# Attention copies by whole units, first scores by pairs, and high parts ahead of low parts in a fused attention, expert and mixer kernel

## What is computed

```python
# 1. attention, 8 heads of 64, 768 positions: window of 16, plus one summary key/value per 32 positions
k_sum = k.reshape(B, H, nb, 32, D).max(axis=3); v_sum = v.reshape(B, H, nb, 32, D).mean(axis=3)
scores = concat([where(|i - j| < 16, q @ k.T, -1e9), q @ k_sum.T + log(32)])   # both scaled by 1/8
x = softmax(scores) @ concat([v, v_sum])
# 2. four experts, each a causal attention of width 64 with an output product; the gate keeps two of them
x = sum over the chosen e of w_e * (softmax(causal(x wq_e (x wk_e).T)) @ (x wv_e)) @ wo_e
# 3. mixer: over tokens (768 -> 256 -> 768), then over channels (512 -> 1536 -> 512), each with a residual
u = x + (relu(x.T @ w_tok1) @ w_tok2).T
out = u + relu(u @ w_ch1) @ w_ch2
```

## Time and profile before

| | |
|---|---|
| median of 3 runs | 444.56 us (444.51 to 444.81) |
| profiled execution | 445.28 us |
| span of its trace | 443.4 us |
| TensorE matmuls busy | 429.9 us, 97% |
| TensorE weight loads busy | 365.1 us, 82% |
| VectorE busy | 294.1 us, 66% |
| ScalarE busy | 228.2 us, 51% |
| GpSimd busy | 144.1 us, 33% |

### The profile page before, as it was taken

The page is one execution under the profiler, slowest core; times in us unless marked ns, Lnnn a source line. Parts: engine busy times, 40 slices in busy tenths (PEclk is TensorE's granted clock), DMA queues, the critical chain, the costliest instruction groups (busy, mean ns, idle before and its releaser), DMA issues.

```text
span 443.4 us, 8595 instructions
## 1 busy us (share of the span) xinstructions
PE 429.9 (97%) x3326; PEld 365.1 (82%) x3326; DVE 294.1 (66%) x531; ACT 228.2 (51%) x592; POOL 144.1 (33%) x162
## 2 busy tenths in 40 slices
PE   7889999999999899999999999999999999999996
PEld 3568996887767799978876898998999898889885
DVE  4885469775469725687766985776775775475353
ACT  5885657765249844876865353444442233323120
POOL 5797947000028602000285265433032022200000
PEclk9999999999999999999999999999999999999999
DMA  8954290000671310000034012123113053301103
GB/s 288 343 200 142 78 316 5 1 2 1 237 294 60 112 58 1 0 1 1 2 96 143 0 49 57 46 88 96 47 49 95 37 201 95 94 3 49 47 1 142
DMA packets 14800, 39.67 MB, mean 89 GB/s; under 512 B 1656, under 2 KB 3368, under 8 KB 14760
## 3 DMA queue, kind: packets, MB, share of 16 engines
q1 hardware_dynamic: 14328, 38.60, 26.2%
q10 hardware_dynamic: 432, 0.52, 0.4%
HBM read 33.56 MB, written 4.72 MB: 86 GB/s over the span
## 4 chain that ended last, share of the span: by engine, by line
PE 87%; DVE 7%; ACT 2%; issue 2%; POOL 1%; DVEq 0%; POOLq 0%
PE ps_s L753 34%; PE ps_o L753 20%; PE ps_x L753 15%; PE ps_t L753 11%; PE ps_t L927 4%; PE ps_t L820 2%; ACT PA L1169 1%; DVE X_l L1569 1%; DVE nmaxA L1432 1%; DVE vsum L1599 1%; DVE PTA L1450 1%; PE ps_x L944 1%; ACT KW L1178 1%; DVE denA L1437 0%; POOL PA L595 0%
## 5 line engine op out<-in xcount | busy, mean ns | idle before, releaser
L1411 ACT ACTIVATE HID_h<-HID_raw 128x384 fp32r<-128x384 f32 x48 | 25.2, 526 | 72.3 <-DVE HID_raw L1768 32.2
L698 POOL TENSOR_TENSOR W_raw<-W_raw 128x256 f32<-128x256 f32 x11 | 11.6, 1055 | 99.9 <-DMA W_raw<-in_ch 88.6
L595 POOL TENSOR_TENSOR PA<-PA,denA 128x480 f32<-128x480 f32 x24 | 23.8, 993 | 51.9 <-DVE denA L1443 51.8
L1169 ACT ACTIVATE PA<-ps_s,nmaxA 128x120 f32<-128x120 f32 x96 | 34.1, 391 | 11.5 <-DVE nmaxA L1432 11.4
L753 PE MATMUL ps_s<-C_h,HID_l 128*128 128x512 f32 x96 | 37.7, 393 | 0.0
L753 PE MATMUL ps_s<-C_l,HID_h 128*128 128x512 f32 x96 | 37.7, 393 | 0.0
L753 PE MATMUL ps_s<-C_h,HID_h 128*128 128x512 f32 x96 | 37.6, 392 | 0.0
L1527 DVE TENSOR_REDUCE nmaxM<-ps_s 128x1 f32<-128x640 f32 (+5 forms) x28 | 26.8, 956 | 13.1 <-PE ps_s L753 13.0
L1757 DVE SCALAR_TENSOR_TENSOR HID_l<-HID_raw,HID_h 128x384 fp32r<-128x384 f32 x48 | 28.1, 590 | 10.5 <-ACT HID_h L1411 8.1
L1239 ACT ACTIVATE PM<-ps_s,nmaxM 128x128 f32<-128x128 f32 (+5 forms) x48 | 30.2, 635 | 5.6 <-DVE nmaxM L1527 5.2
L753 PE MATMUL ps_o<-V_h,W_h 128*128 128x384 f32 x96 | 32.8, 342 | 0.1
(11 more groups left out here) (257 smaller groups left out, 1277.6 us busy)
## 6 DMA issues: line engine op xcount, KB each, us to landing
VW<-in_vw SPq DMA_DIRECT2D x12, 512.0 KB, 7.7
W_raw<-in_ch SPq DMA_DIRECT2D x12, 512.0 KB, 3.6
C_raw<-in_ch SPq DMA_DIRECT2D x12, 512.0 KB, 3.9
VT<-in_vT SPq DMA_DIRECT2D x8, 384.0 KB, 7.3
out_x<-US SPq DMA_DIRECT2D x11, 256.0 KB, 2.0
QT<-in_qT SPq DMA_DIRECT2D x7, 384.0 KB, 7.3
KP<-in_kT SPq DMA_DIRECT2D x6, 384.0 KB, 7.1
raw<-in_tok SPq DMA_DIRECT2D x4, 384.0 KB, 3.2
```

The source lines that it names most:

```text
L595: pool.tensor_tensor(PA[:, u % NPA, :, :], PA[:, u % NPA, :, :], denA[:, u % 2, 1, :].unsqueeze(2).broadcast_to([P, 4, KC]), ALU.mult).the ...
L698: pool.tensor_tensor(W[S3], W[A11], W[A21], ALU.subtract).then_inc(w_sum, 1)
L1169: last = act.activation(PA[:, u % NPA, j, :], ps_s[u % 2][:, j % 2, (j // 2) * KC:(j // 2 + 1) * KC], ACT.Exp, bias=nmaxA[:, u % 4, j:j + ...
L1411: act.activation(*own(s, n, half), ACT.Relu).then_inc(g_hi, 1)
```

## The change

1. A unit's four transposes go into one bank of `ps_t` (bank u % 2), 120x512. ScalarE copies even units, VectorE copies odd units, each in one instruction. The transposes of unit u wait for the copy of unit u-2, the values for one engine's copy.
2. The second means get a function of their own in step 8, in bank 0, behind the copy of unit 4; the transposes of unit 6 wait until they are read. The value sums move to steps 5 and 6. ScalarE writes `VS` from PSUM first, and `VW` from `VS` behind a wait on it.
3. First scores: ScalarE fills pair 0's summary behind its first two window copies, VectorE pair 1's only, reducing pair 0's two halves first. The score matmuls wait pair by pair, behind the mask matmuls. There is one more constant matmul before them (12).
4. `m_out_project` and `m_token1` issue all products with the high part of the moving tile first, wait for the low part only then, and issue the products with it last.
5. The values of unit 0 of batch 1 get a wait of their own for the last `add_tokens` (`m_u`).

```diff
-N_WARM = 11
+N_WARM = 12
-SUMS_AT = (6, 7)
-MEANS_AT = 5
+SUMS_AT = (5, 6)
+MEANS_AT = 8
@@ a_scores
-                if t == 0:
-                    pe.wait_ge(*((a_kfill, 2) if b == 1 and q == 0 else (a_kfill0, 2 * (b + q) + 2)))
+                if t == 0 and b + q > 0:
+                    pe.wait_ge(*((a_kfill, 2) if b == 1 and q == 0 else (a_kfill0, 2 * (b + q) + 1)))
...
                     pair = 2 * q + j
+                    if b + u == 0:
+                        pe.wait_ge(*((a_kfirst, 1) if j == 0 else (a_kfill0, 1)))
@@ a_second_means (new), a_transpose, a_values
+            def a_second_means(b):
+                pe.wait_ge(a_pt0, turned(b, MEANS_AT - 4))
+                means(SECOND_MEANS, b, 1).then_inc(a_vm, 1)
...
-                if u >= 1:
-                    pe.wait_ge(a_pt0, b * NU + u)
-                    pe.wait_ge(a_pt1, b * NU + u)
+                if u >= 2:
+                    pe.wait_ge(a_pt1 if u % 2 else a_pt0, turned(b, u - 2))
+                if u == MEANS_AT - 2:
+                    pe.wait_ge(a_vs, 2 * b + 2)
                 for j in range(4):
-                    last = pe.transpose(ps_t[0:KC, j // 2, (j % 2) * P:(j % 2 + 1) * P], PA[:, u % NPA, j, :], ident[:, :])
+                    last = pe.transpose(ps_t[0:KC, u % 2, j * P:(j + 1) * P], PA[:, u % NPA, j, :], ident[:, :])
...
-                pe.wait_ge(a_pt0, b * NU + (u + 1))
-                pe.wait_ge(a_pt1, b * NU + (u + 1))
+                pe.wait_ge(a_pt1 if u % 2 else a_pt0, turned(b, u))
+                if b > 0 and u == 0:
+                    pe.wait_ge(m_u, b * TQ)
@@ m_out_project
-                pe.wait_ge(m_ol, b * TQ + (t + 1))
+                pe.wait_ge(m_oh, b * TQ + (t + 1))
...
+                for k in range(EP):
+                    mm(ps_x[:, :], OT_h[:, k, :], wo_h[:, k, :], k == 0, False)
+                    mm(ps_x[:, :], OT_h[:, k, :], wo_l[:, k, :], False, False)
+                pe.wait_ge(m_ol, b * TQ + (t + 1))
+                for k in range(EP):
+                    last = mm(ps_x[:, :], OT_l[:, k, :], wo_h[:, k, :], False, k == EP - 1)
@@ m_token1
+                pe.wait_ge(m_xh, b * TQ + (t + 1))
+                cols = slice(m * P, (m + 1) * P)
+                mm(bank[2 * m], tok1_h[:, t, cols], X2_h[:, t, :], t == 0, False)
+                mm(bank[2 * m], tok1_l[:, t, cols], X2_h[:, t, :], False, False)
                 pe.wait_ge(m_xl, b * TQ + (t + 1))
+                last = mm(bank[2 * m], tok1_h[:, t, cols], X2_l[:, t, :], False, t == TQ - 1)
@@ scalar: a_means, a_to_sbuf
+                act.activation(VS[WK:KC, q, :], sums, ACT.Copy, scale=1.0 / BLOCK).then_inc(a_vs, 1)
+                act.wait_ge(a_vs, 2 * b + q + 1)
...
-                act.activation(VW[WK:KC, q, 0:n, :], sums.unsqueeze(1).broadcast_to([NB, n, 2 * P]), ACT.Copy,
-                               scale=1.0 / BLOCK).then_inc(a_vd, 1)
-                act.activation(VS[WK:KC, q, :], sums, ACT.Copy, scale=1.0 / BLOCK).then_inc(a_vs, 1)
+                act.activation(VW[WK:KC, q, 0:n, :], VS[WK:KC, q, :].unsqueeze(1).broadcast_to([NB, n, 2 * P]),
+                               ACT.Copy).then_inc(a_vd, 1)
...
-                act.activation(PTA[:, u % 2, 2:4, :].rearrange("p j q -> p (j q)"), ps_t[0:KC, 1, 0:2 * P],
-                               ACT.Copy).then_inc(a_pt1, 1)
+                act.activation(PTA[:, 0, :, :].rearrange("p j q -> p (j q)"), ps_t[0:KC, 0, :], ACT.Copy).then_inc(a_pt0, 1)
@@ vector: a_to_sbuf, start
-                dve.tensor_copy(PTA[:, u % 2, 0:2, :].rearrange("p j q -> p (j q)"),
-                                ps_t[0:KC, 0, 0:2 * P]).then_inc(a_pt0, 1)
+                dve.tensor_copy(PTA[:, 1, :, :].rearrange("p j q -> p (j q)"), ps_t[0:KC, 1, :]).then_inc(a_pt1, 1)
...
             for r in range(2):
-                half_of_key_maxima(r, 0)
-            for r in range(2):
-                half_of_key_maxima(r, 1)
-                fill_maxima(0, r)
+                for half in range(2):
+                    half_of_key_maxima(r, half)
+            fill_maxima(0, 1)
```

More of the change, by code:

```diff
@@ L278, in program @@
         project_bank = [bank[i][:, 0:GS] for i in (3, 0, 1, 2, 4, 5)] + [ps_o[:, 0:GS], ps_x[:, 0:GS]]
-        FIRST_MEANS = [ps_x[:, 0:2 * P]] + [ps_t[:, 1, 2 * P:4 * P]] * (B - 1)
+        FIRST_MEANS = [ps_x[:, 0:2 * P]] + [ps_t[:, 1, 0:2 * P]] * (B - 1)
+        SECOND_MEANS = ps_t[:, 0, 0:2 * P]
         turn_bank = [ps_o[:, :], ps_x[:, :]]
@@ L308, in program @@
         a_zero = sem("a_zero")
-        a_kfill0 = sem("a_kfill0"); a_kfill = sem("a_kfill")
+        a_kfirst = sem("a_kfirst"); a_kfill0 = sem("a_kfill0"); a_kfill = sem("a_kfill")
         a_kwin0 = sem("a_kwin0"); a_kwin = sem("a_kwin")
@@ L396, in load_half_of_keys, with turned @@
                              kT_d[0, :, r * S + cols.start:r * S + cols.stop]).then_inc((ld_kf, ld_k)[half][r], 16)
+        def turned(b, u):
+            return b * NU // 2 + u // 2 + 1
         def u_row(g, j):
@@ L815, in a_transpose @@
                     pe.wait_ge(a_vs, 2 * b + 1)
-                if u >= 1:
-                    pe.wait_ge(a_pt0, b * NU + u)
-                    pe.wait_ge(a_pt1, b * NU + u)
+                if u >= 2:
+                    pe.wait_ge(a_pt1 if u % 2 else a_pt0, turned(b, u - 2))
+                if u == MEANS_AT - 2:
+                    pe.wait_ge(a_vs, 2 * b + 2)
                 for j in range(4):
-                    last = pe.transpose(ps_t[0:KC, j // 2, (j % 2) * P:(j % 2 + 1) * P], PA[:, u % NPA, j, :], ident[:, :])
-                if u == MEANS_AT:
-                    last = means(ps_t[:, 1, 2 * P:4 * P], b, 1)
+                    last = pe.transpose(ps_t[0:KC, u % 2, j * P:(j + 1) * P], PA[:, u % NPA, j, :], ident[:, :])
                 last.then_inc(a_t, 1)
@@ L868, in m_project @@
                 if g == 4:
-                    pe.wait_ge(a_pt0, b * NU + NU)
-                    pe.wait_ge(a_pt1, b * NU + NU)
+                    pe.wait_ge(a_pt0, turned(b, NU - 2))
+                    pe.wait_ge(a_pt1, turned(b, NU - 1))
                 wh, wl = (wk_h, wk_l) if key else (wq_h, wq_l)
@@ L974, in m_out_project @@
                     pe.wait_ge(m_xn, b * TQ + t)
-                split3(ps_x[:, :], range(EP), lambda k: OT_h[:, k, :], lambda k: OT_l[:, k, :],
-                       lambda k: wo_h[:, k, :], lambda k: wo_l[:, k, :]).then_inc(m_wo, 1)
+                for k in range(EP):
[4 more added lines that the diff above has]
+                    last = mm(ps_x[:, :], OT_l[:, k, :], wo_h[:, k, :], False, k == EP - 1)
+                last.then_inc(m_wo, 1)
             def m_token1(b, t, m):
@@ L982, in m_token1 @@
                     pe.wait_ge(m_exp, b * MU + MU)
+                pe.wait_ge(m_xh, b * TQ + (t + 1))
+                cols = slice(m * P, (m + 1) * P)
+                mm(bank[2 * m], tok1_h[:, t, cols], X2_h[:, t, :], t == 0, False)
+                mm(bank[2 * m], tok1_l[:, t, cols], X2_h[:, t, :], False, False)
                 pe.wait_ge(m_xl, b * TQ + (t + 1))
-                cols = slice(m * P, (m + 1) * P)
-                last = split3(bank[2 * m], [t], lambda k: tok1_h[:, k, cols], lambda k: tok1_l[:, k, cols],
-                              lambda k: X2_h[:, k, :], lambda k: X2_l[:, k, :], t == 0, t == TQ - 1)
+                last = mm(bank[2 * m], tok1_h[:, t, cols], X2_l[:, t, :], False, t == TQ - 1)
                 if t == TQ - 1:
@@ L1033, in sequence @@
                         a_transpose(b, k - 3)
+                    if k == MEANS_AT:
+                        a_second_means(b)
                     if b == 0 and k == 3:
@@ L1317, in sequence @@
                         a_x_hi(b, k - 5)
-                    if 3 <= k <= NU + 2:
+                    if k == MEANS_AT:
+                        a_second_means(b)
+                    if 3 <= k <= NU + 2 and (k - 3) % 2 == 0:
                         a_to_sbuf(b, k - 3)
@@ L1387, in _ @@
             act.activation(mask_m[HALF:P, :, :], mask_m[0:HALF, :, :], ACT.Copy).then_inc(c_rows, 1)
-            for i in range(3):
+            first_windows(0)
+            act.wait_ge(a_ksum, 1)
+            act.activation(KW[:, 0, :, WK:KC], ksum[:, 0, :].unsqueeze(1).broadcast_to([P, NW, NB]), ACT.Copy,
+                           scale=SCALE).then_inc(a_kfirst, 1)
+            for i in range(1, 3):
                 first_windows(i)
@@ L1649, in sequence @@
                         a_maxima(b, k if k < NU else None, k - 1)
-                    if 3 <= k <= NU + 2:
+                    if 3 <= k <= NU + 2 and (k - 3) % 2 == 1:
                         a_to_sbuf(b, k - 3)
```

7 lines of the change are left out of this document (4 added, 3 removed).

## The result

The kernel after takes 440.65 us (four runs, 440.38 to 441.00) beside 444.65 us for the kernel before on the same chip (444.51 to 444.81): a ratio of 0.991, 95% interval 0.9893 to 0.9927. So 4.0 us are gained, where 2.45 were forecast.

A forecast was written before the change was run, and what follows sets the result against it. TensorE held 87% of the chain, but attention steps were taken as bound by VectorE and ScalarE by turns. Gains of 0.2 + 0.5 + 0.5 + 1.25 = 2.45 us from 444.56 gave 442.1 us, range 440.7 to 444.2.

The forecast's parts named there:

- rival D: Start: closing the gap before the first scores raises TensorE's clock earlier, up to 1.4 us gained, 440.7 us; chance 0.13.
- start: First scores by pairs begin near 6.9 instead of 7.10 us: 0.2 us gained, bounds 0 and 0.35.
- attention, both batches: Whole-unit copies, sums and means: 0.5 us gained per batch, bounds 0.3 lost to 1.0 gained, in batch 1 to 1.1.
- high before low: Four places where TensorE waits for a low part, in out-project and token1: 1.25 us gained, bounds 0.6 and 1.7.
- 91.83 and 104.85: Two out-project waits for OT_l in batch 0: 0.2 and 0.4 us gained, as matmuls ahead end near 91.6 and 104.4.
- the 0.5 of out-project 5: Batch 1's end: out-project 5 starts 0.5 us earlier, but this becomes a longer wait for X_l; only 0.46 gained.
- The estimate from the Trainium skill: Whole-unit copies: 0.12 us saved per VectorE pair, 0.14 per ScalarE pair, some 3 us; the forecast counted none of it.
- the maxima of unit 7: Attention, batch 0: both value sums, 0.87 us each, now lie ahead, moving these maxima from 24.13 to about 25.0 us.
- m_value(b, 1): Value projection in attention: limited by unit 7's low part, begins at about 37.15 instead of 37.68 us, 0.5 us gained.
- A: Attention gains nothing and high-before-low works: 443.3 us; chance 0.17.
- B: Neither attention nor high-before-low does much, only batch ends count (0.66 us): 443.9 us, no change; chance 0.12.
- C: Attention: odd steps pay for longer VectorE copies and even steps don't give back; slower, 447.3 us; chance 0.08.

The follow-up runs named there:

- e4_warm12: The kernel before with 12 constant matmuls ahead of the first scores instead of 11, nothing else: 444.64 us, ratio 0.9997.
- e7_outproject: The kernel before with high products first in the out-project alone, token1 as before: 443.01 us, ratio 0.9965.
- e11_x_lo: The kernel after with VectorE's low part of unit 7 ahead of its whole copy of unit 9: 440.20 us, ratio 0.9908 to before.
- e3_start: The kernel before with only the first scores by pairs and the twelfth constant matmul: 444.38 us, ratio 0.999.
- e2_attention: The kernel before with only whole-unit copies, the second means on their own and the earlier value sums: 443.40 us, ratio 0.9969.
- e1_heads: The kernel before with only the high products issued ahead of the low ones, in out-project and token1: 442.57 us, ratio 0.9949.
- e9_token1: The kernel before with high products first in token1 alone: 443.80 us, ratio 0.9978.
- e6_sums_early: The kernel before with nothing but the value sums moved to steps 5 and 6: 444.98 us, ratio 1.0008.
- e12_after_again: The kernel after run once more without an edit: 440.69 us, ratio 0.9906 to before.
- e10_token2: The kernel after with high parts of both tiles before the low parts in the second token product: 440.29 us, ratio 0.9901 to before.
- e5_sums_late: The kernel after with the value sums back at steps 6 and 7: 441.56 us, ratio 0.9936 to before.
- e8_more: The kernel after with high parts first in token2's first two tiles and unit 7's low part ahead of unit 9's copy: 439.81 us, ratio 0.9893 to before.

## Why the prediction was right or wrong

The direction, the three places and their independence were right. All three terms were too small by the medians. The one that moves the time clearly beyond the forecast is the order of the high parts, 2.24 for 1.25. In it and in attention I took what stood behind a wait to be fixed when it could move too. The time itself, 440.65, is next to the 440.7 that I had given to rival D, the clock; that is chance, for D's 1.4 us of clock did not come, as the rivals below show. "In the traces" is after against `e4_warm12`.

| term | forecast | timed alone | in the traces |
|---|---|---|---|
| start | 0.2 (0 to 0.35) | 0.43 | -0.06 at 10 us |
| attention, both batches | 1.0 (-0.6 to 2.1) | 1.41 | 1.28 + 0.34 |
| high before low | 1.25 (0.6 to 1.7) | 2.24 | 1.24 + 1.16 |
| sum | 2.45 | 4.08 | 3.95 |

**High before low: mis-sized by 1.0 us, and beyond its own bounds.** Three steps failed.

1. At 91.83 and 104.85 I priced the waits by where the matmuls ahead end ("they end near 104.4"). These ends are modelled; the queue was free earlier. From start to start, the last transpose ahead and the first product of the out-project are 0.34 and 0.58 us apart in `e4_warm12` and 0.03 in `e7_outproject`, so the gains are 0.33 and 0.56, against 0.2 and 0.4. The second place, timeline of TensorE in `e4_warm12` and then in `e7_outproject`; from the first of the six transposes to the product it is 1.15 us and 0.60:

```profile
102.96 0.85 PE L927 MATMUL ps_t<-ident,PM 128*128 128x128 f32 x6 [0.26 <-issue]
104.11 0.50 PE L753 MATMUL ps_x<-wo_h,OT_h 128*128 128x512 f32 x1 [0.30 <-DVE OT_l L1564]
```

```profile
102.60 0.84 PE L927 MATMUL ps_t<-ident,PM 128*128 128x128 f32 x6 [0.26 <-issue]
103.20 0.48 PE L753 MATMUL ps_x<-wo_h,OT_h 128*128 128x512 f32 x1
```

At the ends of the batches I missed another price. There the first product behind the wait costs 0.34 of the queue (117.60 and 233.88 in `e4_warm12`) and one without a wait 0.23, so the last tile of batch 0 gave 0.35, my 0.2 and this 0.1. At the out-projects behind transposes hardly any of it is saved: the first product costs 0.33 with the wait and still 0.31 without (102.03 to 102.34 in after). I should have read distances from start to start on TensorE, as I did on ScalarE and VectorE.

2. I looked for places with a named wait and missed out-project 4 of batch 1, where before has no bracket, yet waits: from the last transpose to its first product it is 0.19 us in `e4_warm12` and 0.03 in `e7_outproject`, and 0.15 is gained.

3. At the end of batch 1 I let the 0.5 of out-project 5 be lost, because three row sums (the writes of `W_raw`) stand in VectorE's queue ahead of `X_l`. It wasn't lost: 0.54 was gained there and 0.44 at the last tile behind it, where I had 0.46 for both. VectorE's queue is indeed what binds, but an `X_l` of 1.20 us stood further up in that queue, whose like takes 0.68, and once it is short everything behind it moves up. The timeline of after shows the end of it:

```profile
222.23 7.13 POOL L695 TENSOR_TENSOR V_l<-V_raw,V_h 128x256 fp32r<-128x256 f32 x7
225.60 0.69 DVE L1600 TENSOR_TENSOR X_l<-US,X_h 128x512 fp32r<-128x512 f32 x1
232.90 0.68 DVE L1600 TENSOR_TENSOR X_l<-ps_x,X_h 128x512 fp32r<-128x512 f32 x1
233.33 0.39 PE L759 MATMUL ps_s<-X_h,tok_l 128*128 128x512 f32 x1
233.64 0.50 PE L759 MATMUL ps_s<-X_l,tok_h 128*128 128x512 f32 x1
```

The product with `X_l` waits 0.08 us (0.31 from 233.33 instead of 0.23). That this `X_l` is shortened is where GpSimd's instruction happens to stand when VectorE's is issued, so a part of the gain, 0.55 us, is luck of the phase. It came in all eight kernels with the out-project's new order (0.68 or 0.69 in each) and in none of the six without it (1.18 to 1.23), so it is reproducible here, but nothing in the edit secures it. Without it the last `X_l` would come 0.55 later, and as it is what the queue of TensorE waits for there (0.35 us in `e7_outproject`, 0.08 in after), out-project 5's gain would have been lost, as I had said. The Trainium skill ("SBUF — State Buffer", "Who interferes with whom") says that a VectorE instruction with both inputs in SBUF contends with a GpSimd instruction that reads SBUF. The rows agree: `X_l` from `US` takes 0.68 or 1.2 us, `X_l` from `ps_x` 0.68 in all the rows shown, with GpSimd at work beside it.

**Attention: 1.4 instead of 1.0, right in sum, wrong in its parts.** The distances that I took for the copies were right: 0.60 on VectorE, 0.48 on ScalarE for my 0.53. They did not change the sum of work, as said. (The copy at 32.08 in the earlier trace rows that I called the low part's writes the high part, `XT_h`; its 0.26 is right.) The estimate from the Trainium skill ("VectorE: DVE Perf Modes", "The TRN2 errata") of 0.12 and 0.14 us a pair, some 3 us in all, did not come: pairs measured 0.64 against 0.60 and 0.52 against 0.48. The step that failed in batch 0 is that the two sums ahead would move the maxima of unit 7 from 24.13 to about 25.0, and that the means would give back only part of it. The maxima did not move: 23.44 in after, 23.45 in `e4_warm12`. The extra sum of 0.87 fitted in because VectorE's fills shrank (0.80 and 0.49 instead of 0.95 and 0.77), the denominators of unit 5 took 0.16 instead of 0.37, and the copy of unit 0 had left. Why the fills and the denominators were shorter was not tested. So the means' whole 1.2 us was gained rather than 0.6 of it. In batch 1 I foresaw no new wait, and there the 0.87 for GpSimd's key window took back 0.74 of the lead, and the low part of unit 7 took back 0.25 at `m_value(b, 1)`: 0.34 was left, against my 0.5. That `m_value(b, 1)` would be held by the low part of unit 7 behind the longer copy was right, and `e11_x_lo` prices it at 0.1 to 0.23 us in each batch, 0.5 by the medians.

**Start: 0.43 instead of 0.2.** By the median it is a little above its upper bound, though its interval reaches down to 0.04. Against `e4_warm12` the trace of `e3_start` has its first scores 0.34 us earlier, and from the scores of unit 3 on, which wait for the load of `QT`, between 0.14 and 0.21. So the 0.2 was about right for the pairs, and what I gave nothing for is the twelfth constant, 0.17, if that is more than noise. In the trace of after pair 1's fill came late and its scores of unit 2 are not earlier at all: this term differs by some tenths from execution to execution.

**The rivals.** A and B fall with `e2_attention` and `e1_heads`. C, that odd steps pay and even ones don't give back, falls by the time, and in the trace of after, from unit 3 on, VectorE waits for scores only twice: 0.61 us in batch 0, behind the pause at 26.45 of which the last section tells, and 0.43 in batch 1, behind the wait for GpSimd's key window. D, the clock, needs two answers. By the profiles alone it looks right: 1.4 us at 11.4 us between the traces of before and after. But `e1_heads`, `e2_attention` and `e7_outproject` have eleven constants and the old gap before the first scores, and their clock was up before those scores too; and `e4_warm12` keeps its clock over a wait of 0.89 us before them. So closing the gap is not what decides. Before, `e9_token1` and `e6_sums_early` rose late (2.05, 2.08 and 1.91 us for the six constants):

```profile
9.52 2.08 PE L753 MATMUL ps_o<-ident_b 128*128 128x512 bf16 x6
```

(timeline of TensorE in `e9_token1`; 1.47 in after.) So the rise differs from execution to execution of like kernels, and `e4_warm12` prices the constant at 0.17 us in the median. What may be real is the tail. Of 57 runs of before 9 took 445.10 us or more, up to 445.69; of the 22 of `e3_start` and `e4_warm12` none was above 444.82. `e6_sums_early`, with eleven constants, has four in ten at 445.30 or more. Of six profiles with eleven constants three rose late, of eight with twelve none. That is a hint that the constant makes a late rise rarer, not proof. A late rise would also explain the 0.7 us by which the profile of before was slow, since the scores of unit 2 stand 1.5 us later there than in `e4_warm12` and the end 0.8; a comparison of these two single traces alone would have credited the change with 4.7.

## What to carry to other kernels

To price the removal of a wait, read the distance from start to start in the queue, and see what stands ahead of the wait, for that decides whether the first instruction behind it is dearer; modelled ends hide both. A stall isn't tied to the queue behind it just because that queue is long: look in it for instructions that are longer than their likes before you call a gain lost. An edit that does nothing alone can be worth most of a microsecond beside another, when that one frees the place to which it moves the work. And look behind the place for the next wait: the same edit gave 0.31 us in batch 0, and in batch 1 the next wait took it.

## What the runs showed of the hardware

TensorE stood still in the middle of one unit's sixteen small products, with nothing that the profile names as a releaser. In after the pause is 0.72 us, in `e12_after_again` 0.76, in `e11_x_lo` 0.63, in `e10_token2` 0.49, and in `e5_sums_late` and `e8_more` there is none at that place. `e6_sums_early` has one of 0.40 in another unit. In the profiled execution of `e2_attention` it was 1.54 us, and behind it TensorE's granted clock fell, in a kernel that was otherwise at 2.4 GHz. Timeline of TensorE, and then the windows (columns as in the earlier trace rows):

```profile
25.48 0.50 PE L759 MATMUL ps_o<-PTA,VW 120*64 120x64 f32 x9
27.52 0.46 PE L759 MATMUL ps_o<-PTA,VW 120*64 120x64 f32 x7 [1.54 <-issue]
```

```profile
24.00:28.00 4.00, 2.46 (x44) 1.71 (x40) 2.83 (x9) 3.59 (x16) 3.62 (x5) 1.00 0.45 177
28.00:32.00 4.00, 4.00 (x71) 3.23 (x71) 1.55 (x5) 3.17 (x15) 3.38 (x5) 0.65 0.62 169
32.00:36.00 4.00, 4.00 (x70) 3.20 (x70) 2.82 (x9) 3.12 (x15) 2.02 (x3) 0.92 0.52 156
```

After 2.46 us of work in 4, the granted clock was 0.65 in the next four, which is 2.8 of them at 1.2 GHz if only the two levels occur, and the execution took 1.9 us more than the median of its kernel. In after the stretch from 24 to 28 us has 3.28 us of work and the clock stays. Two executions without a trace look alike: 443.38 us of `e11_x_lo` and 443.14 of `e5_sums_late`, 3.2 and 1.6 above their medians, each have a mean granted clock of 0.996 against 0.999 or 1.0 of the others; but so has one of before at an ordinary 444.78, and whether the same pause stood ahead is not known. What makes TensorE pause is open: no wait of the program stands between those products, and I did not try to move it. That the pause brought the clock down is argued from this one execution; if it did, a longer stall in the attention stage costs more than itself.
